# Four of the eight reads of the inverse's blocks moved from SyncE's queue to ScalarE's in every body of the chunk loop

## What is computed

```python
def _attn_ref(q, k, v, beta) -> np.ndarray:
    B, H, S, D = q.shape
    k_n = k / (np.linalg.norm(k, axis=-1, keepdims=True) + 1e-06)
    state = np.zeros((B, H, D, D), dtype=np.float32)
    y = np.zeros_like(q)
    for t in range(S):
        kt, vt, bt = (k_n[:, :, t], v[:, :, t], beta[:, :, t, None])
        y[:, :, t] = np.einsum('bhd,bhde->bhe', q[:, :, t], state)
        v_old = np.einsum('bhde,bhd->bhe', state, kt)
        state = state + bt[:, :, :, None] * np.einsum('bhd,bhe->bhde', kt, vt - v_old)
    return y.astype(np.float32)
...
        h = np.maximum(x[mask] @ w1[e], 0.0)
        ye = h @ w2[e]
        out[mask] = gate_w[mask, None] * eom[mask, e, None] * ye
...
        h = np.maximum(x @ w1[e], 0.0)
        out += p[:, e:e + 1] * (h @ w2[e])
```

## Time and profile before

| what | value |
|---|---|
| median of 3 runs | 1405.78 us |
| lowest and highest | 1403.73 and 1406.74 us |
| the profiled execution | 1409.63 us |
| its span in the trace | 1407.8 us |
| granted PE clock, mean | 0.988 |
| PE, DVE, ACT, POOL busy | 95%, 72%, 26%, 27% of the span |

### The profile page before, as it was taken

How to read it: one execution, slowest core, us unless ns; L and a number is a source line. 1 busy time by engine, 2 the same in 40 slices (tenths; PEclk the granted TensorE clock), 3 DMA queues, 4 the chain that set the end, 5 groups by cost and what they waited for, 6 DMA issues and landing times.

```text
span 1407.8 us, 34320 instructions
## 1 busy us (share of the span) xinstructions
PE 1344.4 (95%) x12765; PEld 1233.6 (88%) x12766; DVE 1016.4 (72%) x1936; ACT 369.0 (26%) x883; POOL 378.2 (27%) x460
## 2 busy tenths in 40 slices
PE   7789899889999999999999999999999999999996
PEld 7789888878999999987999999999999999999995
DVE  5778787656656656678877777777777777777774
ACT  3557667530111111022121111111121111111120
POOL 1001011115444440575122221212131313131325
PEclk8999999999999999999999999999999999999998
DMA  6555554445333321100000000000000000000003
GB/s 145 134 113 136 112 131 111 133 133 184 107 125 107 99 84 62 41 12 13 23 12 22 11 22 11 23 11 22 11 22 11 22 11 22 11 23 11 11 22 112
DMA packets 101967, 85.55 MB, mean 61 GB/s; under 512 B 57520, under 2 KB 93488, under 8 KB 101872
## 3 DMA queue, kind: packets, MB, share of 16 engines
q1 hardware_dynamic: 83232, 51.37, 14.6%
q10 hardware_dynamic: 15568, 23.15, 5.1%
q0 software_dynamic: 3072, 9.71, 1.9%
HBM read 68.01 MB, written 16.18 MB: 60 GB/s over the span
## 4 chain that ended last, share of the span: by engine, by line
PE 85%; DVE 6%; issue 3%; DMA 2%; ACT 2%; SPq 1%; POOL 1%; ACTq 0%; another core or an unknown queue 0%; POOLq 0%; DVEq 0%
PE bank L1034 23%; PE bank L1036 23%; PE bank L1035 23%; PE bank L797 9%; PE bank L1070 2%; PE bank L920 1%; POOL out_dram L791 1%; PE bank L923 1%; ACT R L1228 1%; PE bank L1041 1%; DVE sums L1900 1%; DMA gram_blocks<-R 1%; PE bank L931 1%; DMA kq_sb<-in_kq_dram 1%; DVE terms L1542 0%
## 5 line engine op out<-in xcount | busy, mean ns | idle before, releaser
L1915 DVE SCALAR_TENSOR_TENSOR y_all<-bank,aux_all,y_all 128x384 f32<-128x384 f32 x360 | 217.9, 616 | 107.1 <-PE bank L1036 99.7
L1455 ACT ACTIVATE gTh<-sums 128x512 fp32r<-128x512 f32 x192 | 110.9, 624 | 614.3 <-PE bank L1036 610.6
L1900 DVE TENSOR_TENSOR sums<-bank,sums 128x512 f32<-128x512 f32 x336 | 223.7, 688 | 60.4 <-PE bank L1036 47.1
L1034 PE MATMUL bank<-v2h,gTh 128*128 128x384 f32 x768 | 257.3, 335 | 1.4 <-DVE y_all L1915 0.7
L1036 PE MATMUL bank<-v2h,gTl 128*128 128x384 f32 x768 | 257.2, 335 | 0.0
L1035 PE MATMUL bank<-v2l,gTh 128*128 128x384 f32 x768 | 256.9, 334 | 0.0
L674 POOL TENSOR_TENSOR w_split_sb<-w_raw,w_split_sb 128x384 fp32r<-128x384 f32 (+1 forms) x98 | 110.4, 1170 | 157.0 <-ACT w_split_sb L1409 143.2
L1034 PEld LDWEIGHTS bank<-v2h,gTh 128*128 128x128 f32 x768 | 144.2, 188 | 3.9 <-DVE y_all L1915 1.0
L1035 PEld LDWEIGHTS bank<-v2l,gTh 128*128 128x128 f32 x768 | 144.2, 188 | 1.8
L1036 PEld LDWEIGHTS bank<-v2h,gTl 128*128 128x128 f32 x768 | 144.1, 188 | 0.0
L1904 DVE SCALAR_TENSOR_TENSOR gTl<-sums,gTh 128x512 fp32r<-128x512 f32 x192 | 139.5, 768 | 4.9 <-ACT gTh L1455 1.6
(11 more groups left out here) (239 smaller groups left out, 2714.0 us busy)
## 6 DMA issues: line engine op xcount, KB each, us to landing
w_raw<-in_moe_w_dram ACTq DMA_DIRECT2D x13, 1536.0 KB
xs_in<-x_rows SPq DMA_DIRECT2D x31, 203.0 KB, 2.5
v_raw<-in_moe_w_dram SPq DMA_DIRECT2D x15, 384.0 KB, 3.1
kq_sb<-in_kq_dram SPq DMA_DIRECT2D x28, 192.0 KB, 3.8
kt_sb<-in_kt_dram SPq DMA_DIRECT2D x24, 196.0 KB, 3.0
vt_sb<-in_vt_dram SPq DMA_DIRECT2D x24, 192.0 KB, 3.3
vA_raw<-in_moe_w_dram SPq DMA_DIRECT2D x15, 256.0 KB, 2.6
kq_sb<-in_kq_dram SPq DMA_DIRECT2D x14, 256.0 KB, 5.3
```

What stands on the lines that cost most here:

```text
L1034: pe.matmul(dst, lh, rh, start=first, stop=False)
L1455: act.activation(sum_place(gTh, k), sums[:, SUM_TILE[k]], ACT.Relu).then_inc(g_hi, 1)
L1900: dve.tensor_tensor(out_, x, y, ALU.add).then_inc(sum_ok, 1)
L1915: dve.scalar_tensor_tensor(out=a, in0=src, scalar=share, in1=a, op0=ALU.mult, op1=ALU.add).then_inc(acc_ok, 1)
```

## The change

Before, SP issues all eight reads of chunks 1 to 11. Now SP issues the reads of blocks 4 to 7 and ACT those of blocks 0 to 3, for chunks 2 to 11; chunk 1 is left to SP alone, and chunk 0 is as it was. ACT's four stand at the very end of its body c, for chunk c+2.

```diff
@@ sync engine @@
             def blocks_in(n):
                 sp.wait_ge(inverse_out, 16 * (n + 1))
                 sp.wait_ge(y_clear, n + 1)
-                for u in range(NU // 2 if n == 0 else 0, NU):
+                for u in range(0 if n == 1 else NU // 2, NU):
@@ scalar engine @@
-            def first_in():
-                act.wait_ge(inverse_out, 16)
-                act.wait_ge(y_clear, 1)
+            def blocks_in(n):
+                act.wait_ge(inverse_out, 16 * (n + 1))
+                act.wait_ge(y_clear, n + 1)
                 for u in range(NU // 2):
                     rows, cols = slice(BS * u, BS * u + BS), slice(BS * (u % 4), BS * (u % 4) + BS)
-                    act.dma_start(Y[rows, 0, :, cols], inverse_blocks[0, u].rearrange("h j i -> j h i")).then_inc(y0_in[0], 16)
+                    act.dma_start(Y[rows, n % NY, :, cols], inverse_blocks[n % 2, u].rearrange("h j i -> j h i"))\
+                       .then_inc(y0_in[n % NY], 16)
@@ the end of ACT's body c @@
                 if c >= 1:
                     sums_cleared(c)
+                if c + 2 < NC:
+                    blocks_in(c + 2)
```

More of the change, by code:

```diff
@@ L1325, in _ @@
             level16_rows(0)
-            first_in()
+            blocks_in(0)
             level32_rows(0)
```

## The result

| | before | after |
|---|---|---|
| median | 1406.57 us (8 runs) | 1411.33 us (8 runs) |
| lowest and highest | 1399.13, 1409.61 us | 1408.09, 1415.75 us |
| profiled execution | 1409.63 us | 1413.69 us |
| its span | 1407.8 us | 1411.9 us |
| granted PE clock, mean | 0.988 | 0.982 |

The ratio after to before is 1.004, 95% interval 1.0021 to 1.0059: the change makes the kernel slower by 0.4%, 5.6 us with bounds of 3.0 and 8.3. And it is past the 0.2% that the forecast drew as its limit of "nearly the same".

What follows compares the result with a forecast made beforehand. PE was taken to bound the kernel, idling for late Y and sensitive to ACT's scaling. Pairs +0.6, mean block +2.4 and body 9 -1.5 gave +1.5 us on 1405.78, so 1407.3 us; range 1401.5 to 1413.0.

Steps and rivals of the forecast that it cites:

- What bounds the kernel: PE carries the end; it idles for late Y ahead of `level16_left`, and anything delaying ACT's scaling delays PE equally.
- the case in which ACT's issues cost nothing: Faster rival: PE isn't held by ACT's reads ahead of the scaling; 9.2 us won, 1396.6 us, chance 0.18.
- slower by more than the pairs say: Sign of a wrong forecast: SP's write of the inverse moves later from body to body, dragging everything.
- The pairs of d and I: PE's loss against its gain in each of bodies 1 to 7: 8.3 against 7.7 us, rest +0.6 us.
- d: Delay of PE's second Gram half behind ACT's reads and scaling; 8.3 us over seven bodies with 2.1 us blocks.
- I: PE's idle time ahead of `level16_left`, expected to vanish as Y comes in time; 7.7 us over seven bodies.
- the mean block: ACT's four issues average 2.4 us instead of 2.04, in seven bodies: +2.4 us.
- b: Mean length of ACT's block of four issues; above 2.6 us the kernel is over 0.2% longer.
- SP's spare time elsewhere: SP's four saved issues per body: nothing by the mean, up to 1 us in a body or two.
- Body 9: No scaling follows; PE gets Y in time (1.3 us), the last vt load goes out 1.9 us earlier; together -1.5 us.
- slower through one chain: Rival, chance 0.37: inverse landing, ACT's block, both scalings, blocks of R, next landing; 1411.9 us with 3.05 us blocks.
- both sides nearly cancel: Likeliest case, chance 0.45: PE's gain from early Y and loss at ACT's scaling offset; 1407.3 us, range 1403.0 to 1408.6.

Runs made afterwards that it cites:

- the run with both edits: Kernel before plus ACT's four reads between its two scalings and SP's three kt and kq loads ahead of the blocks of R: ratio 0.9996, 1407.19 us.

## Why the prediction was right or wrong

**What bounds the kernel: right.** Y was late and ACT's slack was in the wrong place. The two rows of waits that the prediction named changed as it said: DVE's 15.6 us became 3.5, and PE's idle time moved from `level16_left` to the second Gram half. Making ACT late with copies alone gave a loss as large as the change's; giving the reads to GpSimd, or to ACT behind the scaling, gave -9.5 us, near the 9.2 us of the case in which ACT's issues cost nothing. The prediction's other sign failed: the transposes were to stay within 0.3 us of their old distance from body to body. Between bodies 1 and 9 they went from 80.39 to 254.12 before and from 79.41 to 262.04 after, 1.1 us more per body. That, with the landing of the inverse later in every body, is what it had named as the sign of "slower by more than the pairs say".

**The pairs of d and I: right.** I was to be 7.7 us, and 1.3 us in body 10; PE's idle time ahead of `level16_left` fell from 9.8 to 0.7, by 9.1. d was to be 8.3 + 2.4 us with the mean block; measured is 11.9 - 0.4 = 11.5. Each sum is off by less than 1 us.

**The mean block: 2.6 us, not 2.4.** The forecast gave b = 2.6 us as the value from which the kernel is over 0.2% slower. The block came out there, which by the forecast's own sum gives +2.8 us; the other 2.8 of the 5.6 us are not in its sum. The two steps that follow are what it left out.

**"SP's spare time elsewhere brings little ... It is nothing by the mean": wrong, and in sign.** I had seen that the second scaling would be late by d and that SP would start on the blocks of R at about the same place. In the trace SP's wait for R went from 4.2 to 35.6 us, and the loads of kq behind the blocks came late for PE, 5.2 us against 0.5. I named what stands behind the waiting instruction on ACT and not what stands behind it on SP. With three loads moved ahead of the blocks these waits are gone and the kernel is 12.6 us faster than the change, so SP's order matters there; what part of the 5.6 us it is isn't shown, as the order may gain by itself. The copies alone, with SP's full queue, lost as much with hardly a wait for kq; so the kq waits are not needed for a loss of that size; the copies kept part of the waits for Y in their place.

**The clock: missing.** The sum priced idle time at its own length. In the change PE ran at 0.96 on the mean in bodies 2 to 9, before at 1.00. Its lower level began at the end of, or right behind, the waits of 1.95 and 2.81 us of body 2, of 2.40 and 1.99 us of body 4, and of 3.60 us of body 6. Over the same matmuls of bodies 2 to 9 this is 3.7 us of busy time beside 5.7 us of idle time in the change, 12.1 beside 12.8 with all eight on ACT, and 1.4 beside 3.6 with the copies, so what goes with the idle time is more than its own length, and not by a fixed factor. Each of these is one execution. The runs of one kernel differ in the same way: of the executions of the kernel before that ran beside the experiments, the seven with a mean clock of 0.981 or 0.982 took 1412.1 us on the mean, the five with 0.990 or 0.991 took 1401.9. The eight of the change had 0.982 on the mean.

**Body 9: the right sign, too small.** The gain of 1.5 us was -3.5 us when taken alone, with an interval that reaches from -6.2 to -0.8. Its half on PE is seen; the wait of ACT for vt stayed at 1 us, which the prediction had named as the sign that its half doesn't come. In the profiled execution of the change body 10 is 1.6 us shorter than before, which is PE's half, and all that stands behind it 2.2 us; with the sharing in bodies 8 and 9 alone it is 1.2 and 4.5 us. Which wait the part behind body 10 is stays open. Body 8 was put at nothing, though PE stood 0.72 us ahead of `level16_left` in body 9 before; 0.69 us of it are still there after, so little was missed.

**The chances.** The case that came, slower through one chain from the landing over ACT's block and both scalings to the blocks of R, had 0.37, with its mechanism and its deciding value named; the likeliest, with 0.45, was that both sides nearly cancel. What separated them were the two terms that the sum left out. That the time lies in the range is in part luck. The upper end was drawn for blocks of 3.05 us, which didn't come, and two errors offset each other: in the profiled executions bodies 2 to 9 lost 9.4 us where the sum has 0.6 + 2.4 = 3.0, and the rest gained 5.3 us where it has 1.5; of these 5.3 us 1.5 lie ahead of body 2, where the start of that stretch differs by more than that between the other runs, and are likely scatter.

## What to carry to other kernels

An engine that idles half its time isn't free at every place: ask what stands behind the moved instruction on that engine, who waits for it, and then the same question again on the queue of who waits. The same shared reads cost 5.6 us with ACT's issues ahead of its scaling and gained 9.4 us with them behind it, where they went out while its ACTIVATEs ran. And two edits that each help can cancel, when one puts large loads in front of small reads that the other has made late.

## What the runs showed of the hardware

- An ACT DMA issue behind ACTIVATEs in the program starts before these have run, 0.28 us after the first of eight had begun, and four of them (0.47 us each) beside a scaling of 1.75 us don't lengthen it. Ahead of ACTIVATEs they hold them for the whole block: one of 3.54 us from 190.19 ended at 193.73, and the scaling started at 193.84.
- Blocks of four such issues took between 1.87 and 3.54 us: in five of the seven bodies one issue took 1.09 to 2.12 us instead of the usual 0.47. SP's four reads into Y, issued at the same time, had one of 1.12 to 1.76 us in the same five bodies and none in the other two.
- GpSimd issued the same plain reads in 0.56 us each.
- A read of 16 KB, by the median 2.7 us from issue to landing in the run with both edits, needed 5.4 us from the end of its issue when it went out among five loads of 190 KB.
- PE's granted clock fell to its lower level behind waits of 1.95 and 2.81 us that lay 3 us apart, and 32 matmuls then took 1.97 us instead of 1.15. A single wait of 2.57 us in the kernel before was followed by no such fall. In bodies 2 to 9 PE was busy for 163.41 us at a mean of 0.96 with the matmuls that took 159.70 us at 1.00.
